# Attention pairs from unit 3 on staged as couples between the steps of the first MLP

## What is computed

```python
for t in range(S):                       # attention, per batch and head
    state = alpha[t][:, None] * state + outer(k[t], v[t])
    y[t] = q[t] @ state
x = y as (3072 tokens, 384)
x = relu(x @ w_in) ** 2 @ w_out          # first MLP, 384 -> 2048 -> 384
out = silu(x @ w2_in)   @ w2_out         # second MLP, other weights
```

## Time and profile before

| | us |
|---|---|
| median of three executions | 874.49 |
| the profiled execution: its own time | 872.96 |
| the profiled execution: span on the core | 871.1 |
| TensorE busy (PE) | 857.6 (98% of the span) |
| VectorE busy (DVE) | 544.1 (62%) |
| ScalarE busy (ACT) | 436.1 (50%) |
| GpSimd busy (POOL) | 106.4 (12%) |

### The profile page before, as it was taken

How to read it: one execution, slowest core, us unless ns; L and a number is a source line. 1 busy time by engine, 2 the same in 40 slices (tenths; PEclk the granted TensorE clock), 3 DMA queues, 4 the chain that set the end, 5 groups by cost and what they waited for, 6 DMA issues and landing times.

```text
span 871.1 us, 17668 instructions
## 1 busy us (share of the span) xinstructions
PE 857.6 (98%) x6834; PEld 708.1 (81%) x6834; DVE 544.1 (62%) x1087; ACT 436.1 (50%) x785; POOL 106.4 (12%) x127
## 2 busy tenths in 40 slices
PE   7999999999999999999999999999999999999998
PEld 6778778888888888888888888888888888888898
DVE  7789877777667667773435556556754446766620
ACT  5765644555445445544567644446434335554410
POOL 3463300000000000000454003003030003000000
PEclk9999999999999999999999999999999999999999
DMA  8884453334333333300412352000230000110010
GB/s 172 233 236 108 101 133 71 82 70 107 76 84 106 75 75 70 104 20 25 158 38 67 60 111 72 0 1 1 53 94 0 1 1 2 36 37 1 1 49 29
DMA packets 134204, 60.04 MB, mean 69 GB/s; under 512 B 81824, under 2 KB 129312, under 8 KB 134112
## 3 DMA queue, kind: packets, MB, share of 16 engines
q1 hardware_dynamic: 130800, 58.14, 27.1%
q10 hardware_dynamic: 3312, 0.69, 0.4%
HBM read 45.02 MB, written 9.44 MB: 63 GB/s over the span
## 4 chain that ended last, share of the span: by engine, by line
PE 95%; DVE 2%; issue 1%; ACT 1%; SPq 1%; DMA 1%; DVEq 0%; ACTq 0%
PE h_ps L1147 22%; PE z_ps L1161 22%; PE h_ps L1190 21%; PE z_ps L1226 11%; PE jobs L1226 7%; PE jobs L1246 3%; PE jobs L1051 1%; PE jobs L1018 1%; PE jobs L1029 1%; PE h_ps L1246 1%; PE h_ps L1124 1%; PE h_ps L1132 1%; DVE decay L1728 1%; PE jobs L1124 0%; PE z_ps L1089 0%
## 5 line engine op out<-in xcount | busy, mean ns | idle before, releaser
L1454 ACT ACTIVATE g<-h_ps 128x512 f32<-128x512 f32 x96 | 57.1, 595 | 160.1 <-PE h_ps L1147 158.0
L1548 ACT ACTIVATE sum<-sum 128x512 f32<-128x512 f32 x96 | 60.5, 630 | 137.8 <-DVE sum L1902 111.4
L1841 DVE TENSOR_TENSOR g_lo<-g,g_hi 128x512 fp32r<-128x512 f32 x96 | 68.7, 717 | 85.9 <-ACT g L1460 85.9
L1902 DVE TENSOR_TENSOR sum<-h_ps,sum 128x512 f32<-128x512 f32 x120 | 82.9, 691 | 57.7 <-PE h_ps L1190 55.1
L1147 PE MATMUL h_ps<-x_hi,win_hi 128*128 128x512 f32 x288 | 114.9, 399 | 2.1 <-DVE x_lo L1833 1.3
L1161 PE MATMUL z_ps<-g_hi,wout_hi 128*128 128x512 f32 x282 | 112.8, 400 | 0.0
L1147 PE MATMUL h_ps<-x_lo,win_hi 128*128 128x512 f32 x288 | 112.3, 390 | 0.0
L1147 PE MATMUL h_ps<-x_hi,win_lo 128*128 128x512 f32 x288 | 112.2, 390 | 0.0
L1161 PE MATMUL z_ps<-g_hi,wout_lo 128*128 128x512 f32 x282 | 110.1, 390 | 0.0
L1161 PE MATMUL z_ps<-g_lo,wout_hi 128*128 128x512 f32 x282 | 110.0, 390 | 0.0
L1190 PE MATMUL h_ps<-s_hi,t_hi 128*128 128x512 f32 x264 | 103.0, 390 | 0.2 <-DVE sum L1902 0.2
(11 more groups left out here) (177 smaller groups left out, 1577.1 us busy)
## 6 DMA issues: line engine op xcount, KB each, us to landing
z_scratch<-z_sb SPq DMA_DIRECT2D x18, 256.0 KB, 2.8
pre<-z_scratch SPq DMA_DIRECT2D x18, 256.0 KB, 3.9
v_sb<-in_v SPq DMA_DIRECT2D x44, 96.0 KB, 2.6
out_x<-z_stage SPq DMA_DIRECT2D x80, 48.0 KB, 1.7
nat_a<-in_alpha SPq DMA_DIRECT2D x40, 88.0 KB, 2.2
nat_k<-in_k SPq DMA_DIRECT2D x40, 88.0 KB, 2.3
nat_q<-in_q SPq DMA_DIRECT2D x40, 88.0 KB, 2.2
nat_a<-in_alpha SPq DMA_DIRECT2D x40, 80.0 KB, 2.3
```

The source lines that it names most:

```text
L1454: nc.scalar.activation(g[f % 2][:], h_ps[f % 2][:], ACT.Relu).then_inc(act_made, 1)
L1548: nc.scalar.activation(at[:], at[:], ACT.Silu).then_inc(silu_made, 1)
L1841: nc.vector.tensor_tensor(low, g[f % 2][:], high.bitcast(F32), ALU.subtract).then_inc(g_lo_made, 1)
L1902: nc.vector.tensor_tensor(to[:], h_ps[(PRODUCTS * n + r) % 2][:], other[:], ALU.add).then_inc(summed, 1)
```

## The change

```diff
+COUPLED = 12
+def coupled(n):
+    return n >= COUPLED
+def beside_others(n):
+    return n != LASTP if coupled(n) else n >= PAIRS and n % PAIRS < PAIRS - 1 and n + 1 != COUPLED
+def sums_first(n):
+    return coupled(n) and n % 2 == 0
+def couple_step(kind, n):
+    first = n - n % 2
+    if first < 16:
+        at = {12: {"A": 27, "KQ": 29, "S": 30, "I": 34, "Y": 35}, 13: {"A": 31, "KQ": 32, "S": 34, "I": 35, "Y": 37},
+              14: {"A": 34, "KQ": 36, "S": 37, "I": 40, "Y": 42}, 15: {"A": 37, "KQ": 38, "S": 40, "I": 42, "Y": 44}}
+        return at[n][kind]
+    base = 4 * first - 20
+    outputs = 4 if base % NF == 12 else 5
+    if n % 2 == 0:
+        return base + {"A": -4, "KQ": -1, "S": 0, "I": 3, "Y": outputs}[kind]
+    return base + {"A": -2, "KQ": 1, "S": 3, "I": outputs, "Y": 7 if n == LASTP else 8}[kind]
 def stage_step(kind, n):
+    if coupled(n):
+        return couple_step(kind, n)
...
 def behind(kind, n):
-    return kind == "I"
+    return kind == "I" and not coupled(n)
...
-    return sorted(jobs, key=lambda j: ("Y", "S", "I", "A", "KQ").index(j[0]))
+    return sorted(jobs, key=lambda j: ("Y", "I", "S", "A", "KQ").index(j[0]))
+def y_slot(n):
+    return 0 if coupled(n) else n % 2
...
-        half_i = (job_ps[2], job_ps[1])
-        half_score = [x[:].rearrange("s b t -> s (b t)")[:, 0:BATCH * HALF] for x in score]
+        def half_i(n):
+            if sums_first(n):
+                return h_ps[(stage_step("I", n) - 1) % 2][:], job_ps[0]
+            return job_ps[2], job_ps[1]
+        def half_score(n):
+            if coupled(n) and n % 2:
+                return [y_tiles[1][:, h * BATCH * HALF:(h + 1) * BATCH * HALF] for h in (0, 1)]
+            return [x[:].rearrange("s b t -> s (b t)")[:, 0:BATCH * HALF] for x in score]
... TensorE, s_stage
-                if n > PAIRS and has_state(n - 1):
+                if n > PAIRS and has_state(n - 1) and not sums_first(n - 1):
                     wait(pe, state_made, n - PAIRS)
... TensorE, i_halves
+                if sums_first(n):
+                    pe.wait_ge(act_made, stage_step("I", n))
+                    pe.wait_ge(y_copied, y_count(n))
... TensorE, y_halves
+                if sums_first(n) and has_state(n):
+                    pe.wait_ge(state_made, n - PAIRS + 1)
... TensorE, ahead of first_product of the next step
                 for kind, n in beside(F - 1):
-                    if kind == "Y" and beside_scores(n):
+                    if kind == "Y" and beside_others(n):
                         pe.wait_ge(y_copied, y_count(n + 1))
+                    if kind == "I" and sums_first(n):
+                        pe.wait_ge(first_added, n - PAIRS + 1)
... ScalarE, y_copy
+                if n > COUPLED:
+                    wait(act, y_moved[(n + 1) % 2], moved((n + 1) // PAIRS, (n + 1) % PAIRS))
... VectorE, a_turn
-                wait(dve, y_made, n - 1)
+                if coupled(n):
+                    wait(dve, kt_made, n - 1)
+                else:
+                    wait(dve, y_made, n - 1)
... VectorE, s_stage
-                wait(dve, y_made, n)
+                wait(dve, y_made, n - 1 if n > COUPLED else n)
+                if n == COUPLED + 1:
+                    wait(dve, y_moved[n % 2], moved(n // PAIRS, n % PAIRS))
... VectorE, the order of a step: ahead of S
+                for kind, n in jobs_here:
+                    if kind == "I" and sums_first(n):
+                        decay_stage(n)
+                        i_stage(n)
                 for kind, n in jobs_here:
                     if kind == "S":
                         s_stage(n)
...
-                    if kind == "I":
+                    if kind == "I" and not sums_first(n):
                         decay_stage(n)
...
-                    if kind == "I":
+                    if kind == "I" and not sums_first(n):
                         i_stage(n)
```

More of the change, by code:

```diff
@@ L152, in outs @@
     return 256 * units if units < UNITS else 256 * (units - 1) + LAST_OUT
-def beside_scores(n):
-    return n >= PAIRS and n % PAIRS < PAIRS - 1
+COUPLED = 12
[16 more added lines that the diff above has]
+    return base + {"A": -2, "KQ": 1, "S": 3, "I": outputs, "Y": 7 if n == LASTP else 8}[kind]
 def stage_step(kind, n):
-    if kind == "Y" and beside_scores(n):
+    if coupled(n):
+        return couple_step(kind, n)
+    if kind == "Y" and beside_others(n):
         return stage_step("S", n + 1)
@@ L292, in build @@
             kp_t = sb("kp_t", [P, BATCH, P], F32, one)
-            y_sb = [sb(f"y_sb{i}", [ROWS, UT], F32, one) for i in range(2)]
+            y_tiles = [sb(f"y_sb{i}", [P, UT], F32, one) for i in range(2)]
             state = sb("state", [ROWS, PAIRS, BATCH, 64], F32, one)
@@ L418, in build @@
         kp = [x[0:ROWS] for x in kp_sb]
+        y_sb = [x[0:ROWS] for x in y_tiles]
         rest = [x[:, 0:SCANS // 2].rearrange("r (b t) -> r b t", b=BATCH)[:, :, 0:P + 1] for x in decay]
@@ L464, in later_y @@
         def later_y(n):
-            return (h_ps[(stage_step("Y", n) - 1) % 2][:] if beside_scores(n) else job_ps[2], job_ps[0])
-        half_i = (job_ps[2], job_ps[1])
-        half_score = [x[:].rearrange("s b t -> s (b t)")[:, 0:BATCH * HALF] for x in score]
+            return (h_ps[(stage_step("Y", n) - 1) % 2][:] if beside_others(n) else job_ps[2], job_ps[0])
+        def half_i(n):
[6 more added lines that the diff above has]
+            return [x[:].rearrange("s b t -> s (b t)")[:, 0:BATCH * HALF] for x in score]
         half_state = [x[0:ROWS].rearrange("s b t -> s (b t)")[:, BATCH * HALF:BATCH * (HALF + HD)] for x in score]
@@ L644, in repack, with repack_halves @@
                     sp.dma_start(x_raw[to:to + n, kk, :], y_sb[p % 2][row:row + n, :]).then_inc(y_moved[p % 2], 16)
-            def repack_halves(p):
+            def repack_halves(pair):
+                p, y = pair % PAIRS, y_sb[y_slot(pair)]
                 for row, kk, to, n in repack_pieces(p):
@@ L649, in repack_halves @@
                     for i, cols in enumerate((slice(0, UT // 2), slice(UT // 2, UT))):
-                        sp.dma_start(x_raw[to:to + n, kk, cols], y_sb[p % 2][64 * i + r:64 * i + r + n, h * UT // 2:(h + 1) * UT // 2]
+                        sp.dma_start(x_raw[to:to + n, kk, cols], y[64 * i + r:64 * i + r + n, h * UT // 2:(h + 1) * UT // 2]
                                      ).then_inc(y_moved[p % 2], 16)
@@ L665, in stage @@
                     wait(sp, y_copied, y_count(n + 1))
-                    repack_halves(n % PAIRS)
+                    repack_halves(n)
                     if more:
@@ L996, in s_stage @@
                 wait(pe, s_copied, 2 * min(n, PAIRS - 1))
-                if n > PAIRS and not beside_scores(n - 1):
+                if n > PAIRS and not beside_others(n - 1):
                     wait(pe, y_copied, y_count(n))
-                if n > PAIRS and has_state(n - 1):
+                if n > PAIRS and has_state(n - 1) and not sums_first(n - 1):
                     wait(pe, state_made, n - PAIRS)
@@ L1050, in i_halves @@
                             tokens = slice(half * HALF, (half + 1) * HALF)
-                            last = nc.tensor.matmul(half_i[half][cols, b * HD:(b + 1) * HD], kp_t[tokens, b, cols],
+                            last = nc.tensor.matmul(half_i(n)[half][cols, b * HD:(b + 1) * HD], kp_t[tokens, b, cols],
                                                     v_tile(n)[tokens, b, h, :], start=True, stop=True, skip_group_check=True)
@@ L1112, in y_halves @@
                     wait(pe, y_copied, y_count(n))
-                if beside_scores(n):
+                if beside_others(n):
                     wait(pe, act_made, stage_step("Y", n))
+                if sums_first(n) and has_state(n):
+                    pe.wait_ge(state_made, n - PAIRS + 1)
                 v_flat = v_tile(n).rearrange("t b h d -> t (b h d)")
@@ L1132, in y_halves @@
                             last = nc.tensor.matmul(out_cols, v_flat[tokens, at:at + cols],
-                                                    half_score[h][tokens, b * HALF:(b + 1) * HALF],
+                                                    half_score(n)[h][tokens, b * HALF:(b + 1) * HALF],
                                                     start=True, stop=True, skip_group_check=True)
@@ L1393, in y_copy @@
                     return
-                if beside_scores(n):
-                    to = y_sb[n % 2][:].rearrange("p (c k t) -> p k c t", c=BATCH, k=2)
+                if beside_others(n):
+                    to = y_sb[y_slot(n)][:].rearrange("p (c k t) -> p k c t", c=BATCH, k=2)
                     for k in (0, 1):
@@ L1401, in y_copy @@
                     return
-                nc.scalar.activation(y_sb[n % 2][:].rearrange("p (c k t) -> p k c t", c=BATCH, k=2),
+                nc.scalar.activation(y_sb[y_slot(n)][:].rearrange("p (c k t) -> p k c t", c=BATCH, k=2),
```

(12 more changed lines are left out.)

## The result

The changed kernel takes 888.0 us (median of five, 886.97 to 890.35) against 874.47 us; the ratio is 1.0164, 95% interval 1.0141 to 1.0187. The forecast was 884.3 us with a range up to 888.5. The median lies just inside; the ratio, put on the forecast's own base of 874.49, gives 888.8 (886.8 to 890.8), just outside. By the ratio the change costs 14.3 us, not 9.8. The direction and the mechanism named for it are there. What was left out is the clock: the profiled execution (890.35 us, span 888.3, the slowest of the five) ran at a mean granted clock of 0.988, and the other four at 0.99, 0.993, 0.991 and 0.993. The profile of before has 1.0.

A forecast was written before the change was run, and what follows sets the result against it. TensorE, busy 98% of the span, was taken to bound the kernel. Stalls of 12.4 us less 2.6 us of saved visits gave 9.8 us more, 884.3 us against the median, range 877 to 888.5.

The forecast's parts named there:

- the mechanism named for it: Steps 44, 52, 60, 68: VectorE finishes KQ late, so TensorE idles 2 to 3.5 us ahead of the scores.
- What bounds the kernel: Steps with attention: TensorE has no idle time, so visits saved and waits added change the time one to one.
- The visits: From step 30 on: 19 TensorE visits instead of 27, eight fewer at 0.33 us, 2.6 us saved (0 to 4.3).
- The stalls: TensorE waits for VectorE at steps 44, 52, 58, 60 and 68, 12.4 us in all (9.4 to 15.4).
- The plain case, A then KQ with nothing else: Steps 58 to 60: VectorE ready for S20 at 11.15 us, TensorE wants it at 9.04; stall 2.1 us.
- The cases behind Y and I: Steps 44, 52, 68: VectorE or relu also delayed by Y and I work; stalls 3.0, 3.4 and 3.4 us.
- the 6.43 us from decay to KQ: Step 42: VectorE's time from the decay through turn, state update and scans to KQ, 6.43 us.
- The clock: TensorE's granted clock stays at 1.00 despite the stalls; no loss taken.
- The third rival: Clock falls to half in the three stalls of 3 us and more: 12.3 us more, 896.6 us; chance 0.04.
- The free edits: First couples' chain, the wait for first_added, the single y buffer and SP's loads: costed at nothing.
- the idle time quoted as a precedent: TensorE idle 1.33 us ahead of pair 9's scores in the old plan, where KQ9 directly follows A9.

The follow-up runs named there:

- e1_spread: Changed kernel with A of pairs 17, 19, 21, 23 at the even pair's scores, KQ of 18, 20, 22 and A20 one step earlier: 870.85 us.
- e7_apart: e1_spread with the sums of odd pairs 13 to 23 put back behind second_product, 25 visits instead of 19: 872.43 us.
- e4_adjacent_alone: Kernel before, uncoupled, with only A of pairs 17, 18, 21, 22 one step later, so KQ follows directly: 889.41 us.
- e2_fill: Changed kernel with 10, 12, 8 and 10 unused matmuls filling TensorE's waits at steps 44, 52, 60, 68: 881.48 us.
- e3_half_fill: Changed kernel with half of e2_fill's unused matmuls (5, 6, 4, 5) ahead of the four waits: 882.19 us.

## Why the prediction missed

**What bounds the kernel: right.** With TensorE full, each us of wait and each visit came through one to one.

**The visits: right, a little small.** The forecast was 2.6 us for eight, 0.33 each; by the starts of e1_spread it is 3.1, 0.39 each, and the six of e7_apart give 0.39 too.

**The stalls: right in place and cause, a little large.** Forecast 3.0, 3.4, 0.5, 2.1, 3.4 at steps 44, 52, 58, 60, 68; measured by starts 2.6, 3.0, 0.7, 2.1, 2.7, so 11.1 for 12.4. The plain case, A then KQ with nothing else, was exact here and 0.15 short in e4_adjacent_alone. The cases behind Y and I were too large because the 6.43 us from decay to KQ came from the earlier trace rows; at step 42 the same chain took 249.17 - 243.14 = 6.03. Most of the difference is VectorE's update, which there could start only when I was through and here found it long done. At step 52 relu of step 50 came 0.93 late, not 1.26, for the same reason.

**The clock: the step that failed.** The prediction said "I take no loss" and gave the fall of the clock a chance of 0.04. It cost 9.1 us of the profiled execution, and some 7 us of the median (e2_fill). Two steps from each stall on, first start to first start, in us; the last line is the difference less the stall:

| steps | 44, 45 | 52, 53 | 60, 61 | 68, 69 |
|---|---|---|---|---|
| changed kernel | 14.65 | 16.40 | 15.58 | 14.62 |
| e1_spread, no stall, clock 1.00 | 10.42 | 10.45 | 10.45 | 10.38 |
| stall by starts | 2.6 | 3.0 | 2.1 | 2.7 |
| left for half clock | 1.6 | 2.9 | 3.0 | 1.6 |

Stalls and visits by themselves would have given 874.5 + 11.1 - 3.1 = 882.5, below the forecast; the clock carried it to the range's end. The third rival named this, with 12.3 us and for stalls of 3 us and more alone. The clock fell behind all four stalls, the one of 2.1 us too, and the price was a third too high: two of the four stretches were short, and a large matmul at half clock takes 0.43 us for 0.23, 1.9 times as long and not twice.

The only evidence against a fall was a misread row. The stretch from 0 to 8 us shows a granted clock of 1.00 after 3.9 us without a matmul, and the changed kernel shows the same above. But the durations of the same instructions on TensorE's timeline of the changed kernel deny it:

```profile
4.77 1.06 PE L1000 MATMUL h_ps<-ident,nat_k 128*112 128x128 f32 x4
6.04 1.10 PE L1000 MATMUL h_ps<-ident,nat_q 128*112 128x128 f32 x4 [0.21 <-DMA nat_q<-in_q]
...
10.17 0.65 PE L1000 MATMUL h_ps<-ident,nat_q 128*112 128x128 f32 x4
...
340.17 1.13 PE L1061 MATMUL jobs<-qp,kp 48*64 48x64 f32 x32 [1.93 <-issue]
341.05 1.08 PE L1072 MATMUL jobs<-ident,kp 48*64 48x48 f32 x32
```

Four transposes take 1.06 to 1.10 us at first and 0.65 from 10 us on. S's groups behind the stall of step 60 (last two rows) take 1.13 and 1.08 us in half clock and 0.69 and 0.66 elsewhere, the same proportion. TensorE was slow at the start, after an idle time, and the clock column did not show it: the trace's first record of the clock stands at 8.88 us (8.16 in the kernel before, whose transposes take 1.06 us at 4.77 and 0.65 at 10.17 as well), and ahead of it the column reads 1.00. The row should have been checked against durations, which would have made the rule of the Trainium skill (TensorE: Matmul & The Clock Gate, "Why this matters for your kernels") the better guide. The trace now agrees with its direction, and gaps shorter than its table names were enough: 1.93 us of idle time between small matmuls at step 60.

**The free edits: right.** The lent bank, first_added, the single y buffer and SP's queue made no wait in any run.

## What to carry to other kernels

Before moving a producer's jobs in a full schedule, add up its chain between the last input that holds it back and the consumer's step; here 11.15 us of VectorE work had 9.04 us, and four numbers in a table turned a gain of 3 us into a loss of 14. On TensorE a stall can cost more than its length, since the clock may fall behind it: here 10.4 us of stalls of 2.1 to 3.0 us took 9.1 us more, and 9.0 us in e4_adjacent_alone 6.3 more. Look for the same fault in the old part of a plan: the idle time quoted as a precedent was worth 1.5 us. And where an effect is smaller than the scatter between executions, compare the starts of the same instructions inside the part that was edited: the spans gave 0.18 us for a visit, the starts 0.39.

## What the runs showed of the hardware

- Idle times of TensorE of 1.93 to 2.84 us between small matmuls were followed by half clock, and four of 2.05 to 2.07 us in e4_adjacent_alone too (0.55 to 0.58 in the stretches above, large matmuls 0.43 us apart instead of 0.23); idle times of 0.81 to 1.25 us in e3_half_fill, and of 1.33 in the earlier trace rows, were not.
- In five executions of the changed kernel the clock's mean went from 0.988 to 0.993, and the time from 890.35 to 886.97 us. Eight to twelve unused matmuls in each gap (e2_fill) gave 1.0.
- One visit of small matmuls fewer, merged with another, saved 0.39 us, the small matmuls being the same in number (e1_spread and e7_apart).
- A granted clock of 1.00 at the start of a trace is no measurement: at 4.8 us four transposes took 1.06 us, at 10.2 us 0.65, with the first record of the clock at 8.88 us.
